# A retention and two-MLP kernel on one core: outputs are copied ahead of decayed values, and the first states are summed pair by pair

## The reference

```python
scores = scale * np.matmul(q, k.transpose(0, 1, 3, 2))
gamma = 1.0 - 2.0 ** (-5.0 - np.arange(H))
Dmat = np.where(rel >= 0, gamma[:, None, None] ** rel[None, :, :], 0.0)   # rel = i - j
x = np.matmul(scores * Dmat[None], v)           # to [4608 tokens, 512]
h = np.maximum(np.maximum(x @ w1, x @ w2), x @ w3)
x = h @ w_out                                    # 512 -> 768 -> 512
h = ((x @ w1) * (x @ w2)) @ w3                   # 512 -> 1024 -> 1024
out = h @ w_out                                  # w3 and w_out are folded to one matrix
```

## Time and profile before

| | us |
|---|---|
| median of 3 timed runs | 1265.27 |
| lowest, highest | 1263.46, 1265.35 |
| the profiled execution, its own time | 1261.15 |
| its span, first to last instruction | 1259.4 |
| TensorE, VectorE, ScalarE, GpSimd busy | 1223.0, 787.4, 486.6, 407.2 |

### The profile page before, as it was taken

The page is one execution under the profiler, slowest core; times in us unless marked ns, Lnnn a source line. Parts: engine busy times, 40 slices in busy tenths (PEclk is TensorE's granted clock), DMA queues, the critical chain, the costliest instruction groups (busy, mean ns, idle before and its releaser), DMA issues. The chain is left out here.

```text
span 1259.4 us, 21123 instructions
## 1 busy us (share of the span) xinstructions
PE 1223.0 (97%) x8288; PEld 1205.0 (96%) x8288; DVE 787.4 (63%) x1198; ACT 486.6 (39%) x771; POOL 407.2 (32%) x216
## 2 busy tenths in 40 slices
PE   6999999999999999999999999999999999899999
PEld 6898889999999999998999999999999999899998
DVE  6877748764646363659698777453535366766563
ACT  3343434422323232325554534242423234455441
POOL 2334218320202020063778571202020117266540
PEclk9999999999999999999999999999999999899999
DMA  9999945020202021053555441313132142344441
GB/s 365 347 350 345 336 144 192 26 101 26 100 26 94 32 82 45 27 175 119 178 197 178 156 154 51 107 51 101 60 103 95 70 174 94 145 156 156 152 157 63
DMA packets 87827, 174.15 MB, mean 138 GB/s; under 512 B 9648, under 2 KB 58416, under 8 KB 87728
## 3 DMA queue, kind: packets, MB, share of 16 engines
q1 hardware_dynamic: 87728, 172.80, 38.7%
HBM read 109.32 MB, written 63.44 MB: 137 GB/s over the span
## 5 line engine op out<-in xcount | busy, mean ns | idle before, releaser
L1026 PE MATMUL ps<-chi,whi 128*128 128x384 f32 x2016 | 676.4, 336 | 15.9 <-DVE wlo L760 8.3
L1028 PE MATMUL ps<-chi,wlo 128*128 128x384 f32 x2016 | 674.7, 335 | 0.0
L1027 PE MATMUL ps<-clo,whi 128*128 128x384 f32 x2016 | 674.6, 335 | 0.0
L551 POOL TENSOR_TENSOR raw<-raw,raw 128x768 f32<-128x768 f32 (+2 forms) x96 | 265.5, 2784 | 592.1 <-DMA raw<-xd 209.7
L1026 PEld LDWEIGHTS ps<-chi,whi 128*128 128x128 f32 x2016 | 379.3, 188 | 21.1 <-issue 10.6
L1027 PEld LDWEIGHTS ps<-clo,whi 128*128 128x128 f32 x2016 | 379.3, 188 | 0.0
L1028 PEld LDWEIGHTS ps<-chi,wlo 128*128 128x128 f32 x2016 | 379.3, 188 | 0.0
L760 DVE TENSOR_TENSOR clo<-raw,chi 128x768 fp32r<-128x768 f32 (+2 forms) x168 | 239.5, 1453 | 24.0 <-ACT chi L683 23.9
L683 ACT CAST chi<-raw 128x768 fp32r<-128x768 f32 (+2 forms) x168 | 180.3, 1081 | 84.7 <-PE ps L1028 59.2
L753 ACT COPY w<-ps 128x384 f32<-128x384 f32 x126 | 60.5, 480 | 229.4 <-PE ps L1028 227.9
L736 ACT COPY u<-ps 128x384 f32<-128x384 f32 x126 | 60.7, 481 | 176.3 <-PE ps L1028 174.9
(11 more groups left out here) (41 smaller groups left out, 847.0 us busy)
## 6 DMA issues: line engine op xcount, KB each, us to landing
qks<-qk SPq DMA_DIRECT2D x32, 576.0 KB, 6.8
gd<-h SPq DMA_DIRECT2D x96, 192.0 KB, 1.9
raw<-gd SPq DMA_DIRECT2D x24, 768.0 KB, 6.0
hd<-h SPq DMA_DIRECT2D x72, 192.0 KB, 1.9
raw<-hd SPq DMA_DIRECT2D x24, 576.0 KB, 5.7
vs<-vv SPq DMA_DIRECT2D x32, 320.0 KB, 7.2
raw<-xd SPq DMA_DIRECT2D x24, 384.0 KB, 5.6
x2d<-h SPq DMA_DIRECT2D x48, 192.0 KB, 2.3
```

Source lines behind the costliest of these rows:

```text
L551: return nc.gpsimd.tensor_tensor(out_, a, b, op)
L1026: nc.tensor.matmul(to, w1, x1, start=(start and k == 0), stop=False, skip_group_check=True)
L1027: nc.tensor.matmul(to, w1, x2, start=False, stop=False, skip_group_check=True)
L1028: last = nc.tensor.matmul(to, w2, x1, start=False, stop=(k == KH[st] - 1), skip_group_check=True)
```

## The change

Three things change; nothing is added or left out, and every engine runs the same number of instructions.

1. ScalarE's step: `read_values` of the read pairs now stands ahead of `decay_values` of the next step's pairs.
2. In step 0, TensorE makes scores 0, sum 0, scores 1, sum 1, and VectorE builds state 0 right behind the decay of scores 0. `make_state(0)` and `make_state(1)` wait for their own sum only.
3. The sum of pair 1 goes to bank 7 (`S_WC`), which the folded weights use from step 3 on, so that VectorE reads bank 6 while TensorE writes sum 1.

```diff
--- before.py
+++ after.py
@@ -691,10 +691,10 @@
                     split_uo(i)
                 if m in WC_READ:
                     read_wc(WC_READ[m])
+                for n in read_in(m):
+                    read_values(n)
                 for n in made_in(m + 1):
                     decay_values(n)
-                for n in read_in(m):
-                    read_values(n)
                 if m in P1_W_HI:
                     split_weight(P1_W_HI[m], 0)
                     split_weight(P1_W_HI[m], 1)
@@ -782,11 +782,12 @@
 
             def make_state(n):
                 p = n % PAIRS
-                dve.wait_ge(state_summed, n + 2 - n % 2)
+                bank = S_WC if n == 1 else S_STATE
+                dve.wait_ge(state_summed, n + 2 - n % 2 if n >= 2 else n + 1)
                 for c in range(NC):
                     for h in range(2):
                         own = slice(h * DH, h * DH + DH)
-                        new = ps[own, S_STATE, (n % 2 * NC + c) * DH:(n % 2 * NC + c + 1) * DH]
+                        new = ps[own, bank, (n % 2 * NC + c) * DH:(n % 2 * NC + c + 1) * DH]
                         if c == 0:
                             nc.vector.tensor_copy(state[n % 2][own, c, own], new).then_inc(state_made, 1)
                         else:
@@ -824,6 +825,8 @@
             for m in range(STEPS):
                 for n in made_in(m):
                     decay_scores(n)
+                    if n == 0:
+                        make_state(n)
                 for n in made_in(m):
                     decay_tail(n)
                 if m in U3_SPLIT:
@@ -835,7 +838,8 @@
                 if m in P1_LO:
                     split_tokens(0, P1_LO[m])
                 for n in made_in(m):
-                    make_state(n)
+                    if n:
+                        make_state(n)
 
             merge = {B: ALU.max, I: ALU.mult}
 
@@ -946,7 +951,7 @@
                         own = slice(h * DH, h * DH + DH)
                         keys = c * P + h * DH
                         at_ = (n % 2 * NC + c) * DH
-                        last = nc.tensor.matmul(ps[own, S_STATE, at_:at_ + DH],
+                        last = nc.tensor.matmul(ps[own, bank, at_:at_ + DH],
                                                 ks[n % 2][:, keys:keys + DH], vdec[n % 2][:, c, own],
                                                 start=(c == 0), stop=(c == NC - 1), skip_group_check=True)
                 last.then_inc(state_summed, 1)
@@ -1001,11 +1006,13 @@
             for m in range(STEPS):
                 for n in made_in(m):
                     scores(n)
+                    if m == 0:
+                        sum_state(n)
                 for i in quarters(m):
                     wc_quarter(i)
                 for n in read_in(m):
                     query_state(n)
-                for n in made_in(m):
+                for n in made_in(m) if m else ():
                     sum_state(n)
                 for n in read_in(m):
                     values(n)
```

## The result

| | before | changed |
|---|---|---|
| median of 7 executions, us | 1264.46 | 1257.76 |
| lowest, highest | 1262.15, 1267.47 | 1256.30, 1260.87 |
| profiled execution, its span | 1259.4 | 1255.2 |

The changed kernel takes 0.9953 of the time, with a 95% interval of 0.9937 to 0.9970. Two more series of the same changed kernel gave 0.9966 (0.9953 to 0.9980) and 0.9959 (0.9945 to 0.9974). Over all series the 25 executions of the changed kernel have a mean of 1257.8 us and the 72 of the kernel before 1263.1: 5.3 us, or 0.4%. The prediction said 1261.1 with a range from 1257.8 to 1264.2: faster is right, and the median, 1257.76, lies on the very low end of the range. The first comparison shows 6.7 us where 4.1 were forecast, the larger sample 5.3.

A forecast was written before the change was run, and what follows sets the result against it. TensorE, busy 97%, was taken as the bound, so only its retention-stage idle time could be won: 1.2 + 1.9 + 1.0 = 4.1 us off the 1265.27 us median gives 1261.1 us, range 1257.8 to 1264.2.

The forecast's parts named there:

- What bounds: Whole kernel: TensorE busy 97%, only its idle time can be won; retention-stage stops for ScalarE's copy, 7.3 us after 20 us.
- Edit 1: First step's sums and states: `query_state` of pair 0 about 2.1 us earlier, 16.5 instead of 18.66; by itself 0 to 2.1.
- Edit 2: ScalarE's copy ahead of `decay_values`: near 34 us copies wait for the `xst` store landing at 35.1; 1.2 us won.
- It keeps up: VectorE's decay of scores 6, about 2.5 us earlier, starts at 36.4, done at 37.6, before `query_state` of pair 4 at 39.9.
- The five later stops: Later TensorE stops for the copy, 3.6 us: four won whole (1.9), the fifth gives 1.0 and keeps about 0.7.
- Decayed values later: `decay_values` behind the copies, 1.2 us later at 37.4; `sum_state` wants it at 41.7, 4.3 us of room, cost nothing.
- C: Rival, chance 0.08: the clock falls in the new gap near 31 to 34 us, about 3 us lost; 1263.2 us.
- The starting number: The median of three timed runs, 1265.27 us, from which the 4.1 us gain was subtracted.
- A: Rival, chance 0.15: stores of `xst` don't hold, landing earlier since the queue is fed earlier; 6.6 us won, 1258.7.
- B: Rival, chance 0.14: DMA engines give back most, each step stops a little at the stores; 1.8 us won, 1263.5.
- D: Rival, chance 0.06: a deeper queue is served at a lower rate, 317 GB/s, below 352; slower, 1268.7 us.
- E: Rival, chance 0.07: scores wait for a second thing at the same moment (q and k loads, tails); nothing moves, 1265.

The follow-up runs named there:

- the eight profiles named above: Eight of ten profiles of kernels with both edits: idle time at 18 us at most 0.7, a wait of 1.0 to 2.5 us near 34.
- the halves alone: Kernel before with ScalarE's new order only, 1258.15 us (0.9958); kernel before with the first step's edit only, 1262.44 us (0.9997).
- the first step's kernel: The changed kernel with ScalarE's old order, leaving the first step's edit and the bank: 1262.44 us, 0.9997 of the kernel before.

## Why the prediction was right, and where not

- **What bounds.** Right. TensorE's stops for the copy went from 7.3 to 2.7 us and the time followed. What was won by the end of the stage, 3.7 us in one pair of profiles, was not lost behind it: the rest is 3.9 ± 0.3 us less.
- **Edit 1, 2.1 us at `query_state` of pair 0.** Wrong by a missed term: 0.7. "VectorE has one state less in front of the decay of pair 2" is true, but that decay waits also for its table of decays, 1.47 us more, and scores 2 and 3 ran at the lower clock (2.08 and 2.05 us instead of 1.41 and 1.12). With the table early, and the clock up by 12.5 us, the 16.5 came out as 16.47. By itself the edit was said to be worth 0 to 2.1 us at 18.66; alone it gives nothing at the end.
- **Edit 2 up to 41 us, 1.2 us.** That the copies there wait for the store of the copy before is right, shown by the rows at 32.93 and 34.43. The size was 1.8: a store issued 1.8 us earlier in the full stretch landed 0.8 earlier, not at the same time, so "issuing earlier doesn't make a transfer land earlier" held for 1.0 of the 1.8 us. But this wait didn't decide what was left at 54 us; VectorE did, as the next point says.
- **"It keeps up."** Right at 39.34, by some 0.3 us, and wrong one step on. The sum had VectorE "about 2.5 us earlier than before" at the decay of scores 6. It was 1.12 us earlier (37.74, not 36.4), because VectorE was not waiting for those scores before: it had worked without a pause since 26.46. The sum also stopped at 37.6 us, ahead of the two low parts, and took no account of GpSimd beside them (0.83 us). The stop at 50 us took most of what stood at 41: 0.5 us were left at 54.
- **The five later stops, 2.9 us.** Nearly right: 3.2 us won after 54 us, 2.7 of them in the stops themselves, and the one stop that was to keep 0.7 us kept 0.71. Two errors of opposite sign, 0.5 instead of 1.2 us in front and 3.2 instead of 2.9 behind, made 3.7 instead of 4.1. That the total came so near is partly luck.
- **Decayed values later, cost nothing.** Right: `sum_state` never waits for them after 20 us.
- **The clock.** It was treated as a risk of the new gap only (C). That gap is 1.6 us in this profile and no fall followed in any of the eight profiles named above. What was missed is the other side: the kernel before loses 5.8 us to the clock on average, and the changed one 1.4 less. That the first step's shorter gap is the reason is not shown: the halves alone lost 5.4 ± 0.5 and 4.6 ± 0.8 us, and the run that filled the early gaps doesn't tell. The section of the Trainium skill that the prediction draws on (TensorE: Matmul & The Clock Gate, Why this matters for your kernels) ties its rule to gaps above a length that 2.69 and 2.64 us don't reach. So those two waits don't go against it, as the prediction said they did.
- **The starting number.** The sum was taken from the median of three, 1265.27; the mean of 72 executions is 1263.1. (1265.27 less 4.1 is 1261.2, not 1261.1.) From the predicted 1261.1 take 2.1 us for the start and 1.4 for the clock, and add 0.2, since the rest went down by 3.9 and not by 4.1: 1257.8, the mean that came out. So the sum's total was nearly right, and the two things beside it made most of the miss.
- **The rivals.** A (stores don't hold) falls by the copies' waits near 34 us, though half of its reason, stores that land earlier, was true for 0.8 us; B (the DMA engines give back) by TensorE's stops for the copy after 54 us, three with 0.9 us; D (a lower rate) by the stretches, 359 GB/s against 352; E by every row above. The span, 1255.2 us against 1255.3, agreed better than its terms did, by luck.

## What to carry to other kernels

Before an instruction is moved forward, list everything that it waits for, and look up when each of these lands, a small table at the end of a queue too: a wait is put down to what came last, and what landed half a microsecond before its reader was ready stands in no list. Follow the second engine as far as the first; if it has no idle time between two of its rows, what is won for the other engine in between is lost at the second. When a copy out of PSUM is freed from what stands ahead of it, the next thing late is the store behind it, and while the DMA engines were full (share 1.04), neither another issuing engine nor a place one load further ahead brought it down sooner here. Compare kernels that differ by a few microseconds with the time lost to the clock taken apart, over many executions, and try to fill the longest gaps of TensorE with spare matmuls whose length is known.

## What the runs showed of the hardware

- A gap does not decide about the clock alone. Waits of 2.77 us were followed by a fall at 591.2 in one profile of the changed kernel and by none in another (at 588.17); waits of 3.38 us were followed by one before the change and by none with the store ahead of v; waits of 2.69 and 2.64 us were followed by none before the change, one of 1.93 us by one in the first step's kernel. Each fall lasts 3.4 or 6.8 us and costs half of it. The Trainium skill (TensorE: Matmul & The Clock Gate, Why this matters for your kernels) says that an idle gap above a certain length between bursts of matmuls drops TensorE to the lower clock; these rows agree for some of the longest gaps and not for others of the same length, and a fall came behind shorter ones too.
- A kernel of 1260 us spreads by 10 us (1257.6 to 1268.2 in 72 executions), more than this whole change; the falls' number is part of it.
- Matmuls of 512 columns in plain fp32 took 0.9 us each, in two records, against 0.26 in fp32r.
- VectorE's subtraction of 128x1024 into fp32r took 1.22 us alone or where it began ahead of GpSimd, and 1.95 to 2.30 where GpSimd's multiplication had begun first. Of two instructions on each engine side by side, the engine that began first took 3.44 us (VectorE) or 3.49 (GpSimd), the other 4.20 to 4.48 (GpSimd) or 4.17 to 4.27 (VectorE).
- In a stretch at 404 GB/s (share 1.04) a store issued 1.8 us earlier landed 0.8 us earlier, and the same store issued by ScalarE landed no sooner.
